# Two of eight weight pieces split inside the first dense stage; first pairs' diagonals, a raw transfer and inverse steps moved

## The reference

```python
for t in range(S):
    y[:, :, t] = np.einsum('bhd,bhde->bhe', rt, state)
    Sa = np.einsum('bhde,bhe->bhd', state, at)
    state_decay = state * wt[:, :, None, :] - np.einsum('bhd,bhe->bhde', Sa, bt)
    state = state_decay + np.einsum('bhd,bhe->bhde', vt, kt)
...
h = x @ w_in            # 320 x 2048
x = (h - np.tanh(h)) @ w_out
...
for e in range(4):      # p: normalized domain_probs
    out += p[:, e:e + 1] * (np.maximum(x @ w1[e], 0.0) @ w2[e])
```

## Time and profile before

| | us |
|---|---|
| median of 3 runs | 1630.55 (1629.51 to 1633.9) |
| the profiled execution | 1631.27 |
| its span | 1629.6 |
| PE busy in the span | 1476.6 (91%) |
| DVE, ACT, POOL busy | 835.4, 397.8, 365.1 |

### The profile page before, as it was taken

The page is one execution under the profiler, slowest core; times in us unless marked ns, Lnnn a source line. Parts: engine busy times, 40 slices in busy tenths (PEclk is TensorE's granted clock), DMA queues, the critical chain, the costliest instruction groups (busy, mean ns, idle before and its releaser), DMA issues.

```text
span 1629.6 us, 37702 instructions
## 1 busy us (share of the span) xinstructions
PE 1476.6 (91%) x15888; PEld 1286.3 (79%) x15888; DVE 835.4 (51%) x1460; ACT 397.8 (24%) x814; POOL 365.1 (22%) x310
## 2 busy tenths in 40 slices
PE   2287687999999999999969999999999999999998
PEld 1266565977877887887858888989989898898887
DVE  7958855967867877765212233333333333332333
ACT  1022233333333333333323222111111111111111
POOL 4121253323323323221234300102020202020000
PEclk9987787999999999999989999999999999999999
DMA  7544585147127326112030220101010101000011
GB/s 180 159 116 124 157 213 148 31 115 195 48 78 198 82 61 176 48 42 58 9 87 18 85 69 1 36 0 36 0 36 0 35 0 35 0 0 0 0 48 48
DMA packets 89417, 112.93 MB, mean 69 GB/s; under 512 B 10952, under 2 KB 67400, under 8 KB 89288
## 3 DMA queue, kind: packets, MB, share of 16 engines
q1 hardware_dynamic: 89288, 111.05, 25.1%
HBM read 78.73 MB, written 32.28 MB: 68 GB/s over the span
## 4 chain that ended last, share of the span: by engine, by line
PE 79%; issue 9%; DVE 4%; POOLq 3%; POOL 3%; DMA 1%; ACT 1%; SPq 0%; DVEq 0%
PE banks L1522 22%; PE banks L1532 21%; PE banks L875 11%; PE banks L884 10%; PE banks L643 2%; POOLq L1299 2%; PE banks L758 1%; PE banks L706 1%; DVE nvmak L1179 1%; PE banks L736 1%; PE banks L723 1%; PE banks L715 1%; PE banks L762 1%; PE banks L616 1%; POOL wo L1321 1%
## 5 line engine op out<-in xcount | busy, mean ns | idle before, releaser
L1522 PE MATMUL banks<-x2t,u 128*128 (+1 forms) x1536 | 380.6, 394 | 0.0
L1532 PE MATMUL banks<-u,hid 128*128 128x320 f32 x2304 | 362.9, 309 | 0.0
L1532 PEld LDWEIGHTS banks<-u,hid 128*128 128x128 f32 x2304 | 350.7, 188 | 13.4 <-issue 0.9
L1626 DVE SCALAR_TENSOR_TENSOR hid<-banks,hid 128x512 fp32r<-128x512 f32 x192 | 132.9, 692 | 408.9 <-ACT hid L1612 408.9
L1522 PEld LDWEIGHTS banks<-x2t,u 128*128 128x128 f32 x1536 | 282.1, 188 | 56.5
L1612 ACT ACTIVATE hid<-banks 128x512 fp32r<-128x512 f32 x192 | 115.0, 599 | 569.1 <-PE banks L1522 569.1
L875 PE MATMUL banks<-xt,wi 128*128 128x512 f32 x768 | 200.1, 404 | 22.2 <-issue 13.3
L884 PE MATMUL banks<-wo,hid 128*128 128x320 f32 x1152 | 183.9, 309 | 5.7 <-POOL hid L1337 5.7
L884 PEld LDWEIGHTS banks<-wo,hid 128*128 128x128 f32 x1152 | 175.4, 188 | 14.2 <-POOL hid L1337 6.4
L875 PEld LDWEIGHTS banks<-xt,wi 128*128 128x128 f32 x768 | 143.8, 193 | 51.0 <-issue 14.8
L1337 POOL TENSOR_TENSOR hid<-shared,hid 128x512 fp32r<-128x512 f32 x96 | 123.7, 1288 | 225.2 <-ACT hid L1036 224.9
(11 more groups left out here) (117 smaller groups left out, 1570.8 us busy)
## 6 DMA issues: line engine op xcount, KB each, us to landing
scaled_operands<-made SPq DMA_DIRECT2D x41, 416.8 KB
made<-kbaw SPq DMA_DIRECT2D x41, 312.0 KB
kb<-scaled_operands SPq DMA_DIRECT2D x24, 416.0 KB
raw<-w SPq DMA_DIRECT2D x8, 640.0 KB, 5.8
lam<-scaled_operands SPq DMA_DIRECT2D x24, 209.6 KB
at<-scaled_operands SPq DMA_DIRECT2D x24, 208.0 KB
raw<-w SPq DMA_DIRECT2D x8, 512.0 KB, 4.0
rt<-rvt SPq DMA_DIRECT2D x96, 40.0 KB
```

The costliest lines, as they stand in the source:

```text
L1522: mm = pe.matmul(self.p_up[f][:], self.u1[:, par, w, f * 128:(f + 1) * 128], self.xt[:, bass.ds(n, 1), x, :].rearrange("p o t -> p (o t)") ...
L1532: mm = pe.matmul(self.p_dn[t][:, 0:D], self.hid[:, f, h, t * 128:(t + 1) * 128], self.u2[:, par, w, f, :], start=(f == 0 and i == 0), stop ...
L1626: dve.scalar_tensor_tensor(out=ex.hid[:, f, 1, :], in0=ex.p_up[f][:], scalar=0.0, in1=ex.hid[:, f, 0, :].bitcast(F32), op0=ALU.max, op1=AL ...
```

## The change

- **Weights.** Pieces 6 and 7 are still loaded in pairs 6 and 7, but split in the first dense stage: in each of the steps f = 1 to 6 of chunk 0, ACT does one of the six copies behind its `hidden_hi(f - 1)`, and POOL one of the six subtractions behind its `hidden_lo(f)`. PE's `up(0, f)` waits at every second f for the piece that it reads.
- **Diagonals.** Those of units 10 and 11 go from pair 1 to the second half of pair 0, where 14 and 15 stand in pair 1. Pair 1 keeps 12 and 13 in its first half.
- **Raw operands** of unit 15 are loaded at the end of SP's pair 0 and no more in pair 1.
- **Inverse of chunk 1.** 8, 28 and 28 steps in pairs 1, 2 and 3 (the places of pair 2: 6, 6, 6, 4, 6 for 4, 6, 6, 4, 8; of pair 3: 6, 6, 6, 4, 6 for 2, 2, 6, 4, 6), and 2 behind pair 3.
- SP waits once more for all pieces ahead of the tokens of chunk 1, which go where piece 6 was.

```diff
 def loaded_in(p):
     if p < 4:
-        return [[], [15], [16, 17], [18]][p]
+        return [[], [], [16, 17], [18]][p]
...
+def pieces_split_in(p):
+    return [i for i, _ in PIECE_PLAN.get(p, []) if i < PIECES - 2]
...
 def diagonals_before(p):
-    return FIRST + sum(len(prepared_in(k)) for k in range(p - 1)) + (2 if p == 2 else 0)
+    return FIRST + sum(len(prepared_in(k)) for k in range(p - 1)) + (2 if p in (1, 2) else 0)
+def first_diagonals(p):
+    return {0: [], 1: [12, 13], 2: []}[p] if p < 3 else prepared_in(p - 1)
+def last_diagonals(p):
+    return {0: [10, 11], 1: [14, 15]}.get(p, [])
...
@@ sync, load_tokens
+                if c == 1:
+                    sp.wait_ge(wi_lo, 4 * PIECES)
@@ sync, pair
                 load_a(p + 2)
                 load_v(p + 2)
+            if p == 0:
+                load_raw(15)
@@ tensor, pair
-            prepared = [] if after_mlp or p == 2 else prepared_in(p - 1)
+            prepared = [] if after_mlp else first_diagonals(p)
+            late = last_diagonals(p)
...
-            for i in prepared[2:3]:
-                diagonal(i)
...
-            for i in prepared[3:]:
-                diagonal(i)
...
-            if p == 1:
-                diagonal(14)
+            for i in late[:1]:
+                diagonal(i)
...
-            if p == 1:
-                diagonal(15)
+            for i in late[1:]:
+                diagonal(i)
@@ tensor, mlp
-            pe.wait_ge(wi_lo, 4 * PIECES)
             pe.wait_ge(xt_lo, 2 * (c + 1))
             for f in range(NF1):
+                if c == 0 and f % W2P == 0:
+                    pe.wait_ge(wi_lo, 4 * (f // W2P + 1))
                 up(c, f)
@@ scalar, pair
-                if b == 1:
-                    for i in prepared[3:]:
+                if b == 2:
+                    for i in last_diagonals(p):
                         save_diagonal(i)
...
-            for i, _ in pieces_in(p):
+            for i in pieces_split_in(p):
                 weight_hi(i)
@@ scalar, mlp
+                if c == 0 and 1 <= f < 7:
+                    weight_hi(PIECES - 2 + (f - 1) // 3, ((f - 1) % 3,))
@@ vector, pair
-            steps = {1: (0, 0, 0, 0, 6), 2: (4, 6, 6, 4, 8), 3: (2, 2, 6, 4, 6)}.get(p, (0, 0, 0, 0, 0))
+            steps = {1: (0, 0, 0, 0, 8), 2: (6, 6, 6, 4, 6), 3: (6, 6, 6, 4, 6)}.get(p, (0, 0, 0, 0, 0))
@@ gpsimd, weight_lo: each part waits for its own copy
-            pool.wait_ge(wi_hi, 3 * (i + 1))
+            for part in parts:
+                pool.wait_ge(wi_hi, 3 * i + part + 1)
@@ gpsimd, mlp
             for f in range(NF1):
                 hidden_lo(c, f)
+                if c == 0 and 1 <= f < 7:
+                    weight_lo(PIECES - 2 + (f - 1) // 3, ((f - 1) % 3,))
```

More of the change, by code:

```diff
@@ L965, in save_natural, with weight_hi @@
                            turn_bank[:, 0:4 * PR].rearrange("p (k e) -> p k e", k=4), ACT.Copy).then_inc(kbn_saved[j], 1)
-        def weight_hi(i):
+        def weight_hi(i, parts=(0, 1, 2)):
             o = spare[:, piece_slot(i), :]
@@ L971, in weight_hi @@
             f = slice(i * W1P, (i + 1) * W1P)
[L972 to L975, removed]
+            if 0 in parts:
+                act.activation(wi[:, HI0:HI1 + 1, f], a[:, 0:2, :], ACT.Copy).then_inc(wi_hi, 1)
+            if 1 in parts:
+                act.activation(wi[:, ST2, f], a[:, 2, :], ACT.Copy).then_inc(wi_hi, 1)
+            if 2 in parts:
+                act.activation(wo[:, 0, i * W2P:(i + 1) * W2P, :],
+                               o[:, 3 * W1P:RAWP].rearrange("p (k d) -> p k d", d=D), ACT.Copy).then_inc(wi_hi, 1)
         def tokens_hi(c):
@@ L995, in pair @@
         def pair(p):
-            prepared = [] if p == 2 or p and drained(p - 1) else prepared_in(p - 1)
+            prepared = [] if p and drained(p - 1) else first_diagonals(p)
             for i in prepared[:1]:
@@ L1001, in pair @@
             save_turned_state(p)
-            for i in prepared[1:3]:
+            for i in prepared[1:]:
                 save_diagonal(i)
@@ L1006, in pair @@
                 save_answer(p, 1, b)
-                if b == 1:
-                    for i in prepared[3:]:
+                if b == 2:
+                    for i in last_diagonals(p):
                         save_diagonal(i)
-                if p == 1 and b == 2:
-                    save_diagonal(14)
-                    save_diagonal(15)
             if p + 1 < NP:
@@ L1308, in decay_state, with weight_lo @@
                                .broadcast_to([PR, 4, PR]), op=ALU.mult).then_inc(state_ready, 1)
-        def weight_lo(i):
+        def weight_lo(i, parts=(0, 1, 2)):
             o = spare[:, piece_slot(i), :]
-            pool.wait_ge(wi_hi, 3 * (i + 1))
             a = o[:, 0:3 * W1P].rearrange("p (k f) -> p k f", k=3)
             f = slice(i * W1P, (i + 1) * W1P)
-            pool.tensor_tensor(out=wi[:, LO0:LO1 + 1, f], in0=a[:, 0:2, :], in1=wi[:, HI0:HI1 + 1, f].bitcast(F32),
-                               op=ALU.subtract).then_inc(wi_lo, 1)
-            pool.drain()
-            pool.tensor_tensor(out=wi[64:128, ST2, f], in0=a[64:128, 2, :], in1=wi[64:128, ST2, f].bitcast(F32),
-                               op=ALU.subtract).then_inc(wi_lo, 1)
-            pool.drain()
-            pool.tensor_tensor(out=wo[:, 1, i * W2P:(i + 1) * W2P, :],
-                               in0=o[:, 3 * W1P:RAWP].rearrange("p (k d) -> p k d", d=D),
-                               in1=wo[:, 0, i * W2P:(i + 1) * W2P, :].bitcast(F32), op=ALU.subtract)\
-                .then_inc(wi_lo, 2)
+            for part in parts:
+                pool.wait_ge(wi_hi, 3 * i + part + 1)
+                if part == 0:
+                    pool.tensor_tensor(out=wi[:, LO0:LO1 + 1, f], in0=a[:, 0:2, :], in1=wi[:, HI0:HI1 + 1, f].bitcast(F32),
+                                       op=ALU.subtract).then_inc(wi_lo, 1)
+                elif part == 1:
+                    pool.drain()
+                    pool.tensor_tensor(out=wi[64:128, ST2, f], in0=a[64:128, 2, :], in1=wi[64:128, ST2, f].bitcast(F32),
+                                       op=ALU.subtract).then_inc(wi_lo, 1)
+                    pool.drain()
+                else:
+                    pool.tensor_tensor(out=wo[:, 1, i * W2P:(i + 1) * W2P, :],
+                                       in0=o[:, 3 * W1P:RAWP].rearrange("p (k d) -> p k d", d=D),
+                                       in1=wo[:, 0, i * W2P:(i + 1) * W2P, :].bitcast(F32), op=ALU.subtract)\
+                        .then_inc(wi_lo, 2)
         def tokens_lo(c):
```

## The result

The changed kernel takes **1611.95 us** (median of 4 runs, 1605.80 to 1616.81), against 1632.22 of the kernel before, run beside it (4 runs, 1629.51 to 1639.29): a ratio of **0.988, with an interval of 0.985 to 0.991**. The forecast was 1610 us, in a range of 1603 to 1619. The profiled execution took 1610.67 us with a span of 1609.0, 20.6 us less than the span before; the forecast took off 20.5.

What follows compares the result with a forecast made beforehand. PE is busy for 91% of the span, so time can be won only where it idles or runs at half clock. -12.6 - 4.6 - 3.3 = -20.5 us, and 0.72 off, from 1631.27 gives 1610 us, range 1603 to 1619.

Steps and rivals of the forecast that it cites:

- Term 1: First dense stage: PE's 8.96 us idle at the entry and the clock fallen behind it go; -12.6 us.
- the 0.8 for DVE's lateness: First dense stage: DVE falls behind by 3 to 4 us by f = 7; 0.8 us lost, between 0 and 3.
- within 1 us: Sign: the first dense stage is as long as the second within 1 us, 62 to 63 us, not 75.
- contention rival: POOL and DVE hold each other up in the dense stage; about 5 us lost, 1615 us; chance 0.10.
- Term 2: Pair 1: unit 15's raw operands come earlier, PE's 3.71 us wait goes, clock gives 2.0, diagonals move; -4.6 us.
- Term 3: Pairs 1 to 3 and behind: inverse steps of chunk 1 moved earlier, eight instructions left of eighteen; -3.3 us.
- the 5 to 7 of the sign: Sign: behind pair 3 PE waits 5 to 7 us for DVE and not 10.9.
- about one step for each POOL instruction: Behind pair 3: on this stretching pattern the eighth inverse instruction ends 8.7 us after the pair; -4.7 us.
- Terms 2 and 3 come to nothing: Rival, pairs 1 to 3: DVE is the bound, only the dense stage counts; 1618 us; chance 0.07.
- It doesn't do what it says: Rival, dense stage: PE still stalls at the entry, `up(0, 12)` or `scores_ur` for 9 us; 1623 us; chance 0.03.
- slower: Rival: the dense stage loses the clock as DVE's lateness makes PE pause; 1647 us; chance 0.03.
- Nothing booked: Pairs 6 and 7: two pieces' copies and subtractions leave ACT and POOL; 0 us booked.

Runs made afterwards that it cites:

- the second profile: The changed kernel run once more, unaltered, against the kernel before; ratio 0.988 (0.986 to 0.991), median 1611.99 us.
- weights alone: Changed kernel with diagonals, raw operands and inverse shares put back as before; pieces 6 and 7 still split in the dense stage; ratio to the kernel before 0.997.

## Why the prediction was right

**Term 1, the weights: right in kind, 1.1 too large.** `up(0, 0)` doesn't wait, and nothing takes its place at the entry; the clock stays at 1.00. The failing number is the 0.8 for DVE's lateness: the stage is 2.0 us longer than the 62.0 of the second, so the sign "within 1 us" missed. `make_gap` is late as foreseen, and latest where I put it: the one wait (287.71) is that of `up(0, 9)`, for `make_gap` of f = 7. But this wait is only a part of the price: the step that has it takes 4.4 us for 3.6. What I left out is that DVE doesn't catch up at once. Each `up` from there to f = 13 starts within 0.3 us behind the `make_gap` that it waits for, and five steps take 3.8 to 3.9 us each (287.71 to 291.62 is the first). That is 0.8 and 1.1 of the 2.0. DVE and POOL in one step f of the changed kernel:

```profile
272.29 1.35 DVE L1141 TENSOR_TENSOR tmp<-tt,ld 128x175 f32<-128x175 f32 x1
273.68 1.59 DVE L1138 TENSOR_TENSOR ld<-ld,tmp 128x175 f32<-128x175 f32 x1
...
275.70 0.36 DVE L1138 TENSOR_TENSOR ld<-ld,tmp 128x192 f32<-128x192 f32 x1
276.09 1.35 DVE L1141 TENSOR_TENSOR tmp<-tt,ld 128x207 f32<-128x207 f32 x1
```

```profile
272.15 1.29 POOL L1361 TENSOR_TENSOR hid<-shared,hid 128x512 fp32r<-128x512 f32 x1 [1.90 <-ACT hid L1053]
273.40 1.67 POOL L1344 TENSOR_TENSOR wo<-spare,wo 128x640 fp32r<-128x640 f32 x1
275.75 1.46 POOL L1361 TENSOR_TENSOR hid<-shared,hid 128x512 fp32r<-128x512 f32 x1 [0.67 <-ACT hid L1053]
```

Each POOL instruction stretches one step, by 1.0 to 1.2 us, as booked. POOL is held up too: 1.46 for 1.29 where a step of DVE was 0.05 us ahead of it, 1.67 for 1.53. The contention rival was thus right in kind, but its 0.4 per POOL instruction measures 0.1 to 0.2, and of its 5 us beyond the forecast term 1 shows 1.1. The Trainium skill ("SBUF — State Buffer", section "SBUF: two separate sides") gives the pair to whoever starts first, and by that rule both engines wait; these rows agree.

**Term 2, raw operands and diagonals: 1.9 too large.** The raw operands came in time and PE's 3.71 us went. The step that failed in this trace is the clock: I took 2.0 us as won, and PEclk was to be 1.00. It was 0.50 from 104 to 112 instead, and DVE waited 4.68 us for PE's right sides of block 3:

```profile
112.61 0.56 DVE L1163 TENSOR_TENSOR rhs<-banks,own 128x160 f32<-128x160 f32 x2 [4.68 <-PE banks L652]
```

The kernel before waited 3.57 at this place, the second profile 2.50, with the clock back some five microseconds earlier; there pair 1 gives 5.5 us up to the transpose and not 3.7, of 6.3 booked. So the clock's part was won in eight of the ten traces, and this is one of the two where it was not. A single trace of before gave its price, and it moves between executions by as much as its own size. (The four numbers of term 2 sum to -4.7; -4.6 was booked.)

**Term 3, the inverse: 4 too small by the table, 1.5 against "weights alone".** Pair 1 (+0.5) and pair 3 (+2.7) are as booked, pair 2 is 1.1 better, which the clock can account for. PE waits 4.91 us behind pair 3, just under the 5 to 7 of the sign. The step that failed is "about one step for each POOL instruction", which gave the tail 8.7 us. DVE's rows of the tail of the changed kernel, with POOL's beside them:

```profile
171.93 2.01 DVE L1141 TENSOR_TENSOR tmp<-shared,ld 128x60 f32<-128x60 f32 x1
173.98 0.22 DVE L1138 TENSOR_TENSOR ld<-ld,tmp 128x60 f32<-128x60 f32 x1
174.23 0.59 DVE L1141 TENSOR_TENSOR tmp<-shared,ld 128x31 f32<-128x31 f32 x1
...
175.09 1.25 DVE L1147 STREAM_TRANSPOSE tt<-ld 128x1024 f32<-128x1024 f32 x1
...
176.84 2.09 DVE L1093 TENSOR_TENSOR_SCAN made<-made 104x128 f32<-104x128 f32 x2
```

```profile
171.72 0.92 POOL L1325 TENSOR_TENSOR st<-st,lam 104x416 f32<-104x416 f32 x1 [0.22 <-issue]
...
172.60 1.26 POOL L1336 TENSOR_TENSOR wi<-spare,wi 128x512 fp32r<-128x512 f32 x1
...
174.02 0.76 POOL L1340 TENSOR_TENSOR wi<-spare,wi 64x256 fp32r<-64x256 f32 x1 [0.16 <-issue]
...
175.00 1.54 POOL L1344 TENSOR_TENSOR wo<-spare,wo 128x640 fp32r<-128x640 f32 x1 [0.22 <-issue]
```

Short steps pass in the gaps, one step waits out two POOL instructions, and the transpose (one operand) keeps its 1.25 us beside the longest of them. The better price is a share of POOL's busy time: before, the tail was stretched by 13.44 - 6.76 = 6.7 us over 8.97 of POOL; with one piece less by 10.94 - 6.76 = 4.2 over 5.3; after, by 5.75 - 3.1 = 2.6 over the 3.9 that don't lie beside the transpose. That is 0.7 to 0.8 of it, in tails of eighteen instructions and of eight. It is a price fitted to these three tails and tested on none. Nor is everything won that the tail no longer shows: POOL's work on piece 2 now lies beside the scan behind it (176.84), which takes 2.09 us where it took 0.73 before. Pair 4 isn't longer for it (18.3 us, before 18.4).

**Rivals.** "Terms 2 and 3 come to nothing" fell: with the old weights they alone give a ratio of 0.994 (0.992 to 0.996), and undoing the inverse costs 4.8 to 7.4 us in the traces. "It doesn't do what it says" and "slower" fell with the entry that no longer waits and the clock of 1.00. "Nothing booked" for pairs 6 and 7 held (-0.2), though the waits in them changed places.

## What to carry to other kernels

Beside a DVE that never rests, price a POOL instruction by its duration, 0.7 to 0.8 of it for steps with both operands in SBUF, and not by a count of steps; then look at what POOL's rest comes to lie beside, since a scan there was stretched as well. Book an idle stretch removed from PE at its length and put what the clock gives back into the range, since one trace shows only one of its values. When two terms of a sum are read from one execution, a total that comes out right doesn't confirm them: lay the same instructions of both traces side by side, stretch by stretch, and do it with a second trace of each kernel before a difference of a few microseconds is given to the code.

## What the runs showed of the hardware

- After PE's idle stretch ahead of the dense stage the granted clock stayed at half for 4 us in one kernel (wait 7.84 us) and for about 9 in another (wait 8.96), with the same products behind it.
- The same code came out between 1605.8 and 1620.1 us over ten executions. The two profiled ones differ by 4.1 us, 2.9 of them by the end of the first dense stage (318.79 and 315.88); the stage itself took 64.0 and 64.1 us. In seven of the eight other runs that leave its order alone it took 64.1 each time; in the eighth, the old shares with one piece less, the clock was at half up to 260.7, in its first `up`, and it took 64.7. What moves most is the recurrence ahead of it, where stretches at half clock fall differently: the same code up to `sides(0)` of pair 4 took 186.3 and 181.0 us, in the kernel before and in "weights alone".
- A DVE step with both operands in SBUF can wait for two POOL instructions that follow without a gap (2.01 and 2.29 us for 0.2 to 0.4). A scan was stretched beside POOL too (2.09 for 0.73), a transpose with one operand was not (1.25). POOL is held up in turn, by 0.1 to 0.2 us.
